# Gate logits computed by token: token blocks stationary, gate weights moving

## The reference

```python
# end of _moe_ref, x is (4, 576, 512)
    gated = u * v_s
    return (x + gated @ w_out).astype(np.float32)      # called x2 in the kernel

# start of _moe2_ref: E = 8 experts, w_gate (512, 8), w_local (512, 1)
    logits = np.einsum('bsd,de->bse', x, w_gate)
    local_gate = 1.0 / (1.0 + np.exp(-np.einsum('bsd,de->bse', x, w_local).squeeze(-1)))
    ...
            fresh_e = int(np.argmax(logits[b, s]))
            if s == 0 or local_gate[b, s] < 0.5:
                e = fresh_e
            else:
                e = prev_e if prev_e >= 0 else fresh_e
```

## Time and profile before

| | us |
|---|---|
| median of 3 runs | 824.75 |
| lowest, highest | 823.78, 825.71 |
| profiled execution: its own time | 827.3 |
| profiled execution: span from first to last instruction | 825.5 |
| PE busy (share of the span) | 758.5 (92%) |
| PEld busy | 643.4 (78%) |
| DVE busy | 454.0 (55%) |
| ACT busy | 345.2 (42%) |
| POOL busy | 197.1 (24%) |
| mean granted TensorE clock | 0.967 |

### The profile page before, as it was taken

The page is one execution under the profiler, slowest core; times in us unless marked ns, Lnnn a source line. Parts: engine busy times, 40 slices in busy tenths (PEclk is TensorE's granted clock), DMA queues, the critical chain, the costliest instruction groups (busy, mean ns, idle before and its releaser), DMA issues.

```text
span 825.5 us, 15547 instructions
## 1 busy us (share of the span) xinstructions
PE 758.5 (92%) x5045; PEld 643.4 (78%) x5046; DVE 454.0 (55%) x877; ACT 345.2 (42%) x750; POOL 197.1 (24%) x371
## 2 busy tenths in 40 slices
PE   4799999999989999999999965699999999999992
PEld 2588888888768988988988945488888888887772
DVE  6688878878535524624623538467273674644221
ACT  2477777777535126116115123245243443351110
POOL 3267887646220000000000000211112112112121
PEclk9999999999999999999999985699999999999997
DMA  6724234322000001001001029616163463311010
GB/s 158 232 57 90 67 72 91 74 66 61 15 16 1 1 1 58 0 0 57 0 0 47 12 85 378 237 44 239 59 231 121 168 234 129 140 40 52 18 51 12
DMA packets 80925, 70.44 MB, mean 85 GB/s; under 512 B 61352, under 2 KB 61352, under 8 KB 80842
## 3 DMA queue, kind: packets, MB, share of 16 engines
q1 hardware_dynamic: 76874, 58.52, 22.8%
q0 software_dynamic: 4000, 11.28, 4.1%
HBM read 59.72 MB, written 11.90 MB: 87 GB/s over the span
## 4 chain that ended last, share of the span: by engine, by line
PE 90%; DVE 4%; issue 2%; ACT 1%; DMA 1%; SPq 1%; POOL 0%; POOLq 0%; ACTq 0%; DVEq 0%
PE sbank L1137 27%; PE sbank L1730 10%; PE sbank L1732 10%; PE sbank L1731 10%; PE tbank L771 5%; PE sbank L800 4%; PE sbank L801 3%; PE obank L847 3%; PE obank L771 3%; PE obank L853 2%; PE obank L1185 2%; PE tbank L1715 1%; PE tbank L1755 1%; PE obank L1755 1%; PE obank L858 1%
## 5 line engine op out<-in xcount | busy, mean ns | idle before, releaser
L1526 POOL DMA_INDIRECT out_dram<-y,sid x25 | 25.3, 1010 | 218.0 <-DVE y L1691 214.7
L1730 PE MATMUL sbank<-w_high,xsT_h 128*128 x184 | 75.3, 409 | 1.9 <-DVE xsT_l L1655 1.7
L1515 POOL COPY gid<-slots 128x1 int32 (+1 forms) x25 | 6.3, 254 | 291.7 <-DVE slots L1415 282.7
L1239 DVE TENSOR_TENSOR w_low<-w_low,w_high (+1 forms) x64 | 74.0, 1218 | 0.7 <-ACT w_high L1595 0.3
L800 PE MATMUL sbank<-k,q 128*128 128x256 f32 (+1 forms) x192 | 72.8, 387 | 0.7 <-ACT probs L579 0.7
L1732 PE MATMUL sbank<-w_low,xsT_h 128*128 x184 | 73.0, 397 | 0.0
L1731 PE MATMUL sbank<-w_high,xsT_l 128*128 x184 | 72.6, 394 | 0.0
L579 ACT ACTIVATE probs<-sbank,nmax 128x128 f32<-128x128 f32 (+3 forms) x128 | 67.2, 536 | 10.9 <-DVE nmax L683 10.9
L1730 PE MATMUL sbank<-w_high,hidT_h 128*128 x176 | 71.0, 404 | 0.2
L1595 ACT CAST w_high<-w_low (+1 forms) x64 | 62.3, 1054 | 16.2 <-SPq L1484 16.2
L1732 PE MATMUL sbank<-w_low,hidT_h 128*128 x176 | 68.8, 391 | 0.0
(11 more groups left out here) (249 smaller groups left out, 1949.1 us busy)
## 6 DMA issues: line engine op xcount, KB each, us to landing
w_low<-in_moe_w_dram SPq DMA_DIRECT2D x16, 2048.0 KB, 13.5
k_raw<-in_k_dram SPq DMA_DIRECT2D x32, 128.0 KB, 2.4
q_raw<-in_q_dram SPq DMA_DIRECT2D x32, 128.0 KB, 2.5
v_raw<-in_v_dram SPq DMA_DIRECT2D x32, 128.0 KB, 2.3
x_dram<-x SPq DMA_DIRECT2D x4, 1024.0 KB, 4.4
win_raw<-in_moe_w_in_dram SPq DMA_DIRECT2D x1, 2048.0 KB, 8.1
wsg_raw<-in_moe_w_sg_dram SPq DMA_DIRECT2D x1, 1152.0 KB, 6.1
wout_raw<-in_moe_w_out_dram SPq DMA_DIRECT2D x1, 1024.0 KB, 10.8
```

Of the source, the lines that this page charges most:

```text
L1239: nc.vector.tensor_sub(w, w.bitcast(F32), piece(w_high, high_place, i).bitcast(F32)).then_inc(wlow_done, 1)
L1730: nc.tensor.matmul(dst, xh, wh, start=first, stop=False)
```

## The change

Stationary and moving operand change places. For each of the five token blocks `t` and each `kk`, the 128x128 piece of x2T is the stationary operand and the 9 columns of `wgate` move; the logits come out by token, 128 partitions by 9, at column 16 t of `obank[:, 0]`, which is just where VectorE's copy L1113 reads them. The signal `logits_turned` now comes from the last of these matmuls. `turn_logits`, ScalarE's copies to `logT`, `logT` itself and two semaphores go. The fifth token block has 64 tokens only, so x2T gets 640 columns instead of 576, and VectorE sets the 64 extra ones of each channel group to zero once (128 partitions by 256 elements) in place of `logT`'s.

```diff
-        x2T = mb("x2T", [P, KT, S], F32)
+        x2T = mb("x2T", [P, KT, SP], F32)
...
-        logT = mb("logT", [E + 1, SP], F32)
...
-        logits_mm = sem("logits_mm")
-        logT_done = sem("logT_done")
...
             def tokens_out(b):
 
-                for n in range(2):
-                    act.wait_ge(logits_mm, 2 * b + n + 1)
-                    nc.scalar.copy(logT[:, halves[n]], obank[0:E + 1, n, 0:HALF]).then_inc(logT_done, 1)
                 act.wait_ge(x2_stored, 16 * (FROM + 2 * b))
...
-            nc.vector.memset(logT[:, S:SP], 0.0).then_inc(pads, 1)
+            nc.vector.memset(x2T[:, :, S:SP], 0.0).then_inc(pads, 1)
...
                 pe.wait_ge(proj_out, 2 * KT * (b + 1))
                 pe.wait_ge(logits_left, FROM + b)
-                for n in range(2):
+                for t in range(ST):
                     for kk in range(KT):
-                        mm = nc.tensor.matmul(obank[0:E + 1, n, 0:HALF], wgate[:, kk, :], x2T[:, kk, halves[n]],
-                                              start=(kk == 0), stop=(kk == KT - 1))
-                    mm.then_inc(logits_mm, 1)
+                        mm = nc.tensor.matmul(obank[:, 0, 16 * t:16 * t + E + 1], x2T[:, kk, P * t:P * (t + 1)],
+                                              wgate[:, kk, :], start=(kk == 0), stop=(kk == KT - 1))
+                mm.then_inc(logits_turned, 1)
...
                     mm.then_inc(x2_turned, 1)
-                    if m == 1:
-                        turn_logits(b)
-
-            def turn_logits(b):
-                pe.wait_ge(logT_done, 2 * (b + 1))
-                stand_alone(pe)
-                for t in range(ST):
-                    mm = nc.tensor.transpose(obank[:, 0, 16 * t:16 * t + E + 1], logT[:, P * t:P * (t + 1)],
-                                             ident[0:E + 1, 0:E + 1])
-                mm.then_inc(logits_turned, 1)
```

## The result

| | us |
|---|---|
| before, median of 4 runs | 825.23 (823.78 to 826.71) |
| after, median of 4 runs | 833.01 (832.59 to 833.57) |
| ratio after / before | 1.0095, interval 1.0075 to 1.0115 |
| profiled execution of after: own time, span | 832.84, 831.1 |

The kernel became slower by 7.8 us. The forecast was 834.0. The forecast's change was +9.3 us on 824.75; the 1.0 us between the two times is smaller than the error of the change because a fourth run raised the median before to 825.23.

A forecast was written before the change was run, and what follows sets the result against it. TensorE, holding 90% of the chain, was taken to bound the kernel. Loads +1.8 us, clock falls +6.0 in three blocks and +1.5 in the last sum to +9.3 on the median 824.75: 834.0 us, range 825.8 to 838.5.

The forecast's parts named there:

- The pairs: New logits, each 128-column load with its 9-column matmul: 0.108 us, paced by the load; +0.44 us per block, +1.8 for four.
- The falls: TensorE's clock falls from 1.00 to 0.50 in or just behind the new logits, in each of the four blocks.
- The price of a fall: Time lost to low clock around the new logits: 2.0 us in each of the first three blocks, 1.5 in the last.
- `L1204` at nothing: Removing the turning of the logits, 0.41 us per block in the chain, was costed as no gain.
- ScalarE's and VectorE's relief at nothing: Dropping ScalarE's logits copies and VectorE's logits copy coming some 1 us earlier were said to gain nothing.
- the memset hidden: VectorE's pad memset grows from 0.11 to an estimated 0.3 us, hidden ahead of an idle stretch of 0.59 us.
- The arithmetic on m = 2: In the x2T transposes, m = 2 must wait for ScalarE's copy of m = 0: 323.19 worked out, 323.20 in the trace.
- B: Rival for the tokens phases: no clock fall, only the load price, 826.5 us (825.9 to 827.2); chance 0.16.
- A: The forecast case: the clock falls in all four blocks, 834.0 us (830 to 838.5); chance 0.62.
- C: Rival for the new logits: a 128-column load is cheaper at full clock, 0.078 us, giving 821.6 us; chance 0.06.
- D: Rival: no clock fall, and the turning's 0.41 us is gained four times, 824.9 us, no change; chance 0.06.

The follow-up runs named there:

- e1: The changed kernel with wgate widened to 96 moving columns per load (9 real, 87 zero): 827.74 us, 1.0029 of the kernel before.
- e9: The kernel before with the changed kernel's 40 pairs (9 columns moving, results unused) added ahead of its logits in each block: 852.13 us, ratio 1.0313.
- e3: e1 with five small transposes, results unused, added between m = 1 and m = 2 of the x2T transposes: 827.69 us, 1.0021 of the kernel before.
- e4: The changed kernel (9 moving columns) with each token block's 8 logits pairs put right ahead of its four transposes: 824.36 us, 0.9984 of the kernel before.
- e7: The kernel before with its logits split into four quarters of 144 tokens in four column groups, four copies to logT: 816.59 us, ratio 0.9893.
- e8: e7 with the four copies to logT moved from ScalarE to VectorE and the turning moved behind m = 3: 814.74 us, 0.9855 of the kernel before.

## Why the prediction was right

- **The pairs: right.** 0.108 us forecast, 0.110 measured at full clock, from `L1462` at half clock and `L838`. Forecast +1.8 us for four blocks; with the clock held (e1) the phases sum to 7.71 + 7.69 + 7.57 + 8.47 = 31.4 us against 7.50 + 7.48 + 7.36 + 8.06 = 30.4, so +1.0 by the traces, and +2.3 by the medians (interval 1.2 to 3.5). The forecast lies in that interval, the traces' 1.0 just under it; where the rest comes from is open. The profiled execution of e1, at 829.94 the slowest of its ten, has low stretches in attention as well (19 to 28 us and 36 to 42.5), where the one of before has none.
- **The falls: right in mechanism and number**, the step on which the forecast rested. The fall after a half busy stretch and the 8.8 us of `L1462` at 0.50 were the evidence; neither shows a fall with TensorE busy throughout, so this was a bet, and the prediction gave it 0.62. e1 has the streaming as the one thing changed, e9 the light pairs as the one thing added, and both bear it out.
- **The price of a fall: near in sum, wrong in where.** Phase of after minus phase of e1: 0.65, 2.30, 2.44 and 1.08 us, 6.5 together; forecast 2.0 three times and 1.5, together 7.5: 1.0 too much. I had spread the low time over the dense stretch behind; in fact it lay on the pairs and the transposes, which it doubles, and the dense stretches lost nothing (55.01, 55.13). In the first block it fell on the transposes alone, whose waits for ScalarE (2.34 us of copies in 3.41) absorbed most of it.
- **`L1204` at nothing: nearly.** It was worth 0.1 us per block (e3), of the 0.41 in the chain. What follows the pairs in the chain shrank from 3.53 us (325.36 - 321.83) to 3.27 in e1 (328.11 - 324.84), so another 0.16 went that I had not seen coming: the first copy on ScalarE starts 0.63 us behind the first transpose instead of 0.69, and the first transposes' loads no longer stand behind a 0.24 us stream. The latter is argued, no run isolates it. So the phases of e1 grew by 0.2 and not by 0.44 in the first three blocks, and the first term of the sum was 0.2 too large in each. The arithmetic on m = 2 took its 0.19 us between copy and transpose from m = 4; in e1, m = 2 starts 0.10 us behind the copy's end (325.31 + 0.54 = 325.85; TensorE at 325.95) and m = 4 (327.38) again 0.19 behind its own. Only m = 4 has a `stand_alone` (a semaphore raised by TensorE itself) in front, a likely reason that no run isolates. By the traces the loads' term is 0.8 too large in all and the falls' 1.0: 7.5 in place of 9.3, two small errors the same way.
- **ScalarE's and VectorE's relief at nothing, the memset hidden: right.** The logits' copy comes 1 us earlier, counted from the start of the phase, and the routing waits for the exponentials as before; the new memset (228.13, 0.27 us) ends 0.38 us before VectorE is released.
- **Rivals.** B (no fall) is what e1 is: 827.74, in place of the 826.5 worked out for it; the changed kernel itself had the four falls of A. The rule of the Trainium skill that stood for B (TensorE: Matmul & The Clock Gate, "What's actually happening": an idle stretch lets the clock fall) is too narrow here: none of the four falls in `tokens` has an idle TensorE ahead of it. C fell with 0.110 us, D with e3.

What is left: the profiled executions differ by 5.6 us in span, the medians by 7.8. The phases alone account for 37.91 - 30.40 = 7.5 us. Before's profile has a low stretch at 262.34 that after's does not have, and after's a longer one around 231; the profiles of the experiments have the one or the other too, and I did not try to separate it.

## What to carry to other kernels

Swapping stationary and moving operand so that few columns move turns a stream into weight loads: cost it by the loads (here 0.11 us per plain fp32 load of 128 columns, whatever moves up to 96), and then ask what it does to the clock, which here fell because too little streamed while the engine was busy without a gap. If a small product has to be on the path, keep the narrow operand stationary and put pieces of the stream into different column groups (3.98 to 1.10 us here), then look at which copies were free only because the product was slow. An entry of the chain that stands in front of a double-buffered step (the 0.41 us of the turning) is worth what is left after the buffer's own wait, here 0.1.

## What the runs showed of the hardware

- 48 zero-padded columns per load left the clock falling in two of four blocks of the profiled execution, 96 in none; the padding was zeros, so columns that move hold the clock even where their values are zero. Why one block and not another falls with 48, or with e4's mixture, was not settled.
- Four column groups with 144 plain fp32 columns each ran nearly fully side by side: 32 records in 1.14 us, where 16 of 288 columns had taken 3.98 (a quarter of that is 1.00), and the clock held (e7, e8), although TensorE waits for 0.6 to 0.8 of some 5 us in the first three phases of e7.
- A low stretch on the path cost 0.65 us of its 3.41 where it lay on transposes with waits for ScalarE in between, and 2.3 to 2.4 of 6.83 where pairs were in it as well; dense matmuls lose more, 1.4 of 3.41 (16 records in place of 27).
- fp32 transposes brought the clock up. In the first block of after TensorE ran nothing else from 321.47 to 324.88, at 0.50, and the clock was 1.00 from then on; in the second block likewise from 386.32 to 389.73. Pairs with 50 moving columns never did so in 8.8 us (`L1462`).
